# Attention, one expert layer and a gated FFN on one core: token numbers copied in FFN units, SP's order of a step, turn counts read by pairs, third row group used from unit 12

## The reference, cut to what matters

```python
def phi(x):
    proj = np.einsum('bhsd,df->bhsf', x, w_phi)
    proj = proj - np.max(np.abs(proj), axis=-1, keepdims=True)
    return np.concatenate([np.exp(proj), np.exp(-proj)], axis=-1)
# attention, batch 4, 8 heads, 576 positions, head size 64
kv = einsum(phi(k), v); z = sum(phi(k)); x = (phi(q) @ kv) / (phi(q) @ z + 1e-6)
# 2304 tokens of 512, top-1 of 8 experts, hidden 1024
e = argmax(x @ w_gate); y = gate_w * eom * (relu(x @ w1[e]) @ w2[e])
# gated FFN, hidden 1536
xn = y / sqrt(mean(y * y) + 1e-6) * rms_g
out = (silu(xn @ w_gate) * (xn @ w_val)) @ w_out
```

## Time and profile before

| | us |
|---|---|
| three runs | 873.22, 875.22, 879.47; median 875.22 |
| the profiled execution, its own time | 873.63 |
| span of its profile | 871.9 |
| PE busy | 840.2 (96% of the span) |
| DVE busy | 538.9 (62%) |
| ACT busy | 347.3 (40%) |
| POOL busy | 161.4 (19%) |
| mean granted TensorE clock | 0.998 of full speed |

### The profile page before, as it was taken

One profiled execution on the slowest core, in us unless ns is written; L12 is line 12 of the kernel. 1 busy time (PEld: TensorE's weight loads), 2 busy tenths in 40 slices (PEclk: granted clock), 3 DMA queues, 4 the chain that ended last, 5 costly groups with the idle time before them and its releaser, 6 DMA issues.

```text
span 871.9 us, 16594 instructions
## 1 busy us (share of the span) xinstructions
PE 840.2 (96%) x6216; PEld 757.3 (87%) x6217; DVE 538.9 (62%) x934; ACT 347.3 (40%) x547; POOL 161.4 (19%) x169
## 2 busy tenths in 40 slices
PE   8999999998988999999989999999999999999997
PEld 6685867767988999999989999999999998888885
DVE  5688786989766954445569777666765774212210
ACT  4544454573155533322354443333433443212211
POOL 1010302112350433203421031111110000101101
PEclk9999999999999999999999999999999999999999
DMA  8613713112349544554662852232421945343320
GB/s 285 209 57 138 275 54 108 55 38 75 127 175 267 227 114 97 141 148 150 184 230 77 280 180 79 79 80 79 142 71 54 357 150 184 123 139 125 125 101 36
DMA packets 65226, 122.41 MB, mean 140 GB/s; under 512 B 9200, under 2 KB 43120, under 8 KB 62480
## 3 DMA queue, kind: packets, MB, share of 16 engines
q1 hardware_dynamic: 57600, 91.98, 34.3%
q0 software_dynamic: 3488, 17.85, 5.3%
q10 hardware_dynamic: 4080, 11.80, 3.9%
HBM read 77.54 MB, written 44.09 MB: 139 GB/s over the span
## 4 chain that ended last, share of the span: by engine, by line
PE 78%; DVE 11%; issue 6%; DMA 2%; ACT 1%; DVEq 1%; SPq 0%; another core or an unknown queue 0%; POOLq 0%; POOL 0%; ACTq 0%
PE ps L1207 9%; PE ps L1209 9%; PE ps L1208 9%; PE ps L1259 5%; PE ps L1258 5%; PE ps L1260 5%; PE ps L956 3%; PE ps L1115 3%; PE ps L1116 3%; PE ps L1117 3%; PE ps L1128 3%; PE ps L1130 3%; PE ps L1129 3%; PE ps L1011 3%; PE ps L916 2%
## 5 line engine op out<-in xcount | busy, mean ns | idle before, releaser
L1207 PE MATMUL ps<-sH,tb 128*128 128x384 f32 x504 | 171.0, 339 | 5.9 <-DVE val L2018 2.9
L1208 PE MATMUL ps<-sL,tb 128*128 128x384 f32 x504 | 170.0, 337 | 0.0
L1209 PE MATMUL ps<-sH,tb 128*128 128x384 f32 x504 | 169.9, 337 | 0.0
L1207 PEld LDWEIGHTS ps<-sH,tb 128*128 128x128 f32 x504 | 95.0, 189 | 8.5 <-DVE val L2018 4.9
L1208 PEld LDWEIGHTS ps<-sL,tb 128*128 128x128 f32 x504 | 95.1, 189 | 0.1
L1209 PEld LDWEIGHTS ps<-sH,tb 128*128 128x128 f32 x504 | 95.2, 189 | 0.0
L2036 DVE TENSOR_TENSOR hTL<-h_st,hTH 128x768 fp32r<-128x768 f32 x36 | 33.0, 954 | 97.4 <-ACT hTH L1516 97.4
L1260 PE MATMUL ps<-woH,hTL 128*128 128x512 f32 x216 | 84.1, 389 | 0.0
L1259 PE MATMUL ps<-woL,hTH 128*128 128x512 f32 x216 | 84.1, 389 | 0.0
L1258 PE MATMUL ps<-woH,hTH 128*128 128x512 f32 x216 | 84.0, 389 | 0.0
L1115 PE MATMUL ps<-xmH,w1H 128*128 128x288 f32 x256 | 76.8, 300 | 5.9 <-issue 2.8
(11 more groups left out here) (246 smaller groups left out, 1784.8 us busy)
## 6 DMA issues: line engine op xcount, KB each, us to landing
h_dram<-hid SPq DMA_DIRECT2D x36, 384.0 KB, 2.8
h_st<-h_dram SPq DMA_DIRECT2D x18, 768.0 KB, 4.1
t_dram<-tb SPq DMA_DIRECT2D x6, 1792.0 KB, 5.7
t_raw<-in_ffn_up SPq DMA_DIRECT2D x13, 512.0 KB, 3.2
tb<-t_dram ACTq DMA_DIRECT2D x6, 1024.0 KB, 6.7
xin<-xs_dram SPq DMA_DIRECT2D x9, 578.2 KB, 9.3
xs_dram<-zrow SPq DMA_DIRECT2D x8, 578.2 KB, 7.9
qT<-in_q SPq DMA_DIRECT2D x4, 1152.0 KB, 5.8
```

The source lines that it names most:

```text
L1207: e.matmul(to, wh, xh, start=(fresh and c == 0), stop=False, skip_group_check=True)
L1208: e.matmul(to, wh, xl, start=False, stop=False, skip_group_check=True)
L1209: done = e.matmul(to, wl, xh, start=False, stop=(c == 1), skip_group_check=True)
```

## The change

1. **Token numbers.** The copies to `ids_dram` leave the steps of the expert stage. All eight are issued by SP in the FFN units 6, 8, ..., 20 (a loop in unit 21 takes further steps, of which there are none with these inputs). `idF` is read in unit 23 and not 15, `idI` made in unit 25 and not 17.
2. **SP's order of a step.** `rows_out` stands before `step_weights_in`.
3. **SP's order at the turn to the FFN.** `group_in(0)` comes before `operands_in(0)`; `operands_in(1)` waits for DVE's first copy of group 0 (`s_hi0`) and no more for PE's last hidden chunk. In unit 4 the last rows' store and `group_in(2)` stand before `hidden_out(4)`.
4. **Turn counts.** The two numbers of both turns are read at the pair's beginning; DVE reads the first TILES of the next pair there too.
5. **Third row group.** Visit 5 of groups 0 and 1 moves ahead; group 2 is first used at unit 12 and not 10. Its sums are made by DVE in units 9 "B", 10 "A" and 10 "B"; its splits move by two units. Visit 6's weights are split in unit 14 and not 13. Each group's sums have a semaphore of their own.

```diff
-MADE_AT = {6: 13, 7: 16, 8: 19, 9: 22, 10: 23, 11: 26}
-UNITS = ([(v, sg) for sg in range(2) for v in range(3)] + [(3, 0), (3, 1), (4, 0), (4, 1), (3, 2), (4, 2)]
-         + [(v, sg) for v in range(5, 9) for sg in range(NSG)]
+MADE_AT = {6: 14, 7: 16, 8: 19, 9: 22, 10: 23, 11: 26}
+UNITS = ([(v, sg) for sg in range(2) for v in range(3)] + [(v, sg) for v in range(3, 6) for sg in range(2)]
+         + [(v, 2) for v in range(3, 6)] + [(v, sg) for v in range(6, 9) for sg in range(NSG)]
...
+SUM_AT = {(1, "A"): ((1, 0), (1, 1)), (1, "B"): ((1, 2), (1, 3)), (9, "B"): ((2, 0), (2, 1)), (10, "A"): ((2, 2),),
+          (10, "B"): ((2, 3),)}
...
+NUMBERS_AT = tuple(range(6, 6 + 2 * (NTOK // G), 2))
...
-        def turn_of(e, x):
-
-            tiles = e.value_load(tab[0:1, bass.ds(x + TILES, 1)], min_val=0, max_val=NTOK // G)
-            first = e.value_load(tab[0:1, bass.ds(x + FIRST, 1)], min_val=0, max_val=NTOK // G + E)
-            return tiles, first
+        def turns_of(e, pair):
+
+            return [(e.value_load(tab[0:1, bass.ds(pair * 2 + (par + TILES), 1)], min_val=0, max_val=NTOK // G),
+                     e.value_load(tab[0:1, bass.ds(pair * 2 + (par + FIRST), 1)], min_val=0, max_val=NTOK // G + E))
+                    for par in range(2)]
...
             with e.Fori(0, pairs) as pair:
-                for par in range(2):
-                    tiles, first = turn_of(e, pair * 2 + par)
+                counts = turns_of(e, pair)
+                for par, (tiles, first) in enumerate(counts):
...
             with e.Fori(0, total - 2) as n:
                 rows_next(n + 2)
                 weights_out(n + 1)
+                rows_out(n, column_of(n))
                 step_weights_in(n + 2)
-                col, row = column_of(n), row_of(n)
-                rows_out(n, col)
-                numbers_out(n, col, row)
...
-            e.wait_ge(s["e_st"], 16 * 8)
-            operands_in(0)
             e.wait_ge(s["xst"], total * 16)
             settle(e, "carry_sp")
             group_in(0)
-            prior_col, prior_row = column_of(prior), row_of(prior)
-            rows_out(prior, prior_col)
-            e.wait_ge(s["pe_s1"], total * FC)
-            settle(e, "carry_sp")
+            e.wait_ge(s["e_st"], 16 * 8)
+            operands_in(0)
+            rows_out(prior, column_of(prior))
+            e.wait_ge(s["s_hi0"], 1)
             operands_in(1)
...
             for u in range(NU):
-                hidden_out(u)
                 if u == ROOT_AT + 1:
                     rows_out(last, last_col)
                     e.wait_ge(s["s_lo"], 7)
                     e.wait_ge(s["xst"], total * 16 + 32)
                     settle(e, "carry_sp")
                     group_in(2)
+                hidden_out(u)
...
-                if u == 8:
-                    numbers_out(prior, prior_col, prior_row)
-                if u == 10:
-                    numbers_out(last, last_col, last_row)
-                if u == 15:
-                    e.wait_ge(s["idst"], total * 16 + 16)
+                if u in NUMBERS_AT:
+                    n = NUMBERS_AT.index(u)
+                    if n > 0:
+                        e.wait_ge(s["idst"], n * 16)
+                    with nc.allow_non_contiguous_dma(reason="token numbers"):
+                        e.dma_start(ids_dram[bass.ds(column_of(n), G), :], xs_dram[bass.ds(row_of(n), G), DM:DM + 1])\
+                            .then_inc(s["idst"], 16)
...
             e.wait_ge(s["s_lo"], 7)
             add_squares(total - 1)
-            e.wait_ge(s["s_lo"], 14)
-            row_sums(2, 0)
-            row_sums(2, 1)
...
                 with e.Fori(0, pairs) as pair:
-                    for par in range(2):
-                        tiles, first = turn_of(e, pair * 2 + par)
-                        nxt = e.value_load(tab[0:1, bass.ds(pair * 2 + (par + TILES + 1), 1)], min_val=0,
-                                           max_val=NTOK // G)
+                    counts = turns_of(e, pair)
+                    after_pair = e.value_load(tab[0:1, bass.ds(pair * 2 + (TILES + 2), 1)], min_val=0, max_val=NTOK // G)
+                    for par, (tiles, first) in enumerate(counts):
+                        nxt = counts[1][0] if par == 0 else after_pair
...
             def beside(u, pos):
 
+                for sg, n in SUM_AT.get((u, pos), ()):
+                    row_sum(sg, n)
```

More of the change, by code:

```diff
@@ L307, in build_program @@
             "FFN up weights of a step: loaded, sums, operands split, stored": "e_in e_add e_hi e_lo e_st",
-            "FFN rows loaded (one per group), their sums, operands split": "x_in0 x_in1 x_in2 s_add s_add1 s_hi0 s_hi s_lo",
+            "FFN rows loaded (one per group), their sums, operands split": "x_in0 x_in1 x_in2 s_add0 s_add1 s_add2 s_hi0 s_hi s_lo",
             "FFN up operands loaded (two parts per buffer)": "t_a0 t_a1 t_a2 t_b0 t_b1 t_b2",
@@ L579, in rows_next, with numbers_out @@
                 rows_in(row)
-            def numbers_out(n, col, row):
-                e.wait_ge(s["idst"], n * 16 + 16)
+            def numbers_out(n):
+                e.wait_ge(s["idst"], n * 16)
                 settle(e, "carry_sp")
                 with nc.allow_non_contiguous_dma(reason="token numbers"):
-                    e.dma_start(ids_dram[bass.ds(col, G), :], xs_dram[bass.ds(row, G), DM:DM + 1])\
+                    e.dma_start(ids_dram[bass.ds(column_of(n), G), :], xs_dram[bass.ds(row_of(n), G), DM:DM + 1])\
                         .then_inc(s["idst"], 16)
@@ L669, in _ @@
             operands_in(2)
-            last_col, last_row = column_of(last), row_of(last)
+            last_col = column_of(last)
             for u in range(NU):
-                hidden_out(u)
                 if u == ROOT_AT + 1:
@@ L681, in _ @@
                         weights_in(vis)
-                if u == 8:
-                    numbers_out(prior, prior_col, prior_row)
-                if u == 10:
-                    numbers_out(last, last_col, last_row)
-                if u == 15:
-                    e.wait_ge(s["idst"], total * 16 + 16)
+                if u in NUMBERS_AT:
+                    n = NUMBERS_AT.index(u)
+                    if n > 0:
+                        e.wait_ge(s["idst"], n * 16)
+                    with nc.allow_non_contiguous_dma(reason="token numbers"):
+                        e.dma_start(ids_dram[bass.ds(column_of(n), G), :], xs_dram[bass.ds(row_of(n), G), DM:DM + 1])\
+                            .then_inc(s["idst"], 16)
+                if u == NUMBERS_AT[-1] + 1:
+                    with e.If(total > NTOK // G):
+                        with e.Fori(NTOK // G, total) as n:
+                            numbers_out(n)
+                if u == NUMBERS_AT[-1] + 3:
+                    e.wait_ge(s["idst"], total * 16)
                     settle(e, "carry_sp")
@@ L2099, in _ @@
                 beside(u, "C")
-                if u == 17:
+                if u == NUMBERS_AT[-1] + 5:
                     e.wait_ge(s["id_in"], 16)
```

62 lines of the change are left out of this document (26 added, 36 removed).

## The result

The changed kernel takes 879.83 us (median of 20 runs, 876.48 to 884.87). The kernel before, run beside it on the same chip, takes 876.86 us (20 runs, 873.22 to 879.72). The ratio is 1.0033, with a 95% interval of 1.0019 to 1.0047: about 3 us slower. That is within 1% as forecast, but on the other side of 1, and the time is over the range's end of 877.5. The profiled execution of the changed kernel has a span of 877.0 us.

The account below looks back on a forecast made before the run. PE, busy 191.0 of 198.8 us in the expert stage, leaves only gaps, some 9 us touched. Terms +2.2 + 1.5 - 1.8 - 4.0 + 2.0 - 1.5 + 0.2 = -1.4 from 873.6 give 872.2, stated as 872.0; range 866 to 877.5.

Parts of the forecast that it names:

- Part 4: FFN unit 4: its store, behind the rows' store and group 2's load, delays unit 6's sigmoid; +2.0 us.
- "very late" rival: Unit 4: rows' store held behind both ACT loads to about 502, unit 4's store lands near 512; 875.3 us, chance 0.13.
- The second landing: Unit 4's store, issued at 501.0 behind group 2's load, lands 9.2 us later, at 510.2.
- The upper bound: Unit 4's store: at most a 3.6 us gap of PE plus a fall of the clock.
- The rule that I weighed against the rows: DMA engines alternate between queue rows packet by packet, so unit 4's store would come in time; sum 2 us lower.
- Part 2: Expert steps: the rows' store goes out 3.7 us earlier, ending PE's 1.83 us wait for ACT's copy; -1.8 us.
- Part 3: Turn to the FFN: group 0's load first removes PE's 0.60 and most of 2.52 us, and the clock's fall; -4.0 us.
- Part 1: Expert stage: reading four counts at a pair's start lengthens two gaps by 1.44 us, removes 0.71 between turns; +2.2 us.
- The clock's fall behind the 3.1 us gap: First pair's start: a gap forecast at 3.0 us drops PE's clock to half; +1.5 us, chance 0.6.
- Part 5: FFN units 8 to 10: moving the third group's sums from POOL to DVE removes unit 9's 1.54 us gap; -1.5 us.
- Part 6: Smaller edits: unit 14's weight splits may delay ACT by some tenths, plus chance hits of POOL's sums; +0.2 us.
- the base: The profiled execution's own 873.6 us, from which the terms were counted; the three runs' median is 1.6 higher.

Follow-up runs that it names:

- f1: The changed kernel itself, measured again on another chip: 870.78 us against 870.04 before, ratio 1.0004.
- f2: The changed kernel with unit 4's store back ahead of the last rows' store and group 2's load, on f1's chip: 863.35 us, ratio 0.9922.
- e2: The kernel before with only unit 4's store moved behind the last rows' store and group 2's load: 882.71 us against 875.01, ratio 1.0089.
- e3: The kernel before with only both turns' counts read at a pair's start: 876.86 us against 875.01, ratio 1.0021.
- e8: The changed kernel with unit 4's store between SP's wait for the last rows' landing and group 2's load: 872.17 us against 878.28 before, ratio 0.9934.
- e11: The kernel before with only the token numbers' copies moved out of the expert steps, old order of rows' store and weights' load: 866.31 us, ratio 0.9955.
- e4: The kernel before with only the turn to the FFN changed (group 0 loaded first, second visit's operands later): 873.84 us against 875.01, ratio 0.9983.
- f3: The changed kernel with unit 4's store first and counts read turn by turn as before, on f1's chip: 863.86 us, ratio 0.9925.
- e1: The changed kernel with unit 4's store back ahead of the last rows' store and group 2's load: 869.25 us against 875.01 before, ratio 0.9932.

## Why the prediction was wrong

*Part 4, the store of unit 4, forecast +2.0, measured 7.4 (f1 against f2) and 7.7 (e2).* This is the step that failed: the chain of waits, its place and the instruction that waits were right, the size was not. The step that was wrong is "the store landed 6.4 us after its issue: 500.3". The 6.4 us of the earlier trace rows were taken as what the store needs, and kept while its issue moved 3.3 us forward. But it was mostly a wait for ACT's loads, whose time SP's order doesn't change. Before, ACT's second load was issued at 493.33 and the rows' store at 496.85, 3.5 us behind it; now the distance is 0.8 us (492.81 and 493.59), no packet of the store moved before 497.5, and it took 8.4 us. An issue 3.3 us earlier brought a landing only 1.2 us earlier (503.2 and 502.0), and the whole list behind it went out 1.7 us later than forecast. The four runs with unit 4's store behind the rows' store have 8.4 to 9.1 us there; of the other twelve runs and the kernel before, all have 6.1 to 7.4, but for e3's 9.7. With that unit 4's store landed at 512.1, which is the "very late" rival almost to the tenth, by its own reason (the rows' store held back behind ACT's loads to about 502); I gave it 0.13. The second landing, 9.2 us behind group 2's load, was right (9.4). And the rival itself was priced too low, with a gap of 3.6 (measured 4.19) and one fall of the clock of 1.5 us; the clock stayed at half for twice as long, which cost some 2.5. The upper bound should have been about 8, not 5.

What stands behind a load on SP's own queue waited for it: 9.4 us against 4.4 in e8. The rule that I weighed against the rows (Trainium skill, DMA: Bandwidth & Descriptors, "Queues, rings and completion order", queue rows take turns packet by packet) is about transfers of different queue rows, and spoke for the rows' store beside ACT's loads. The trace doesn't bear out what I drew from it: from 494.2 to 497.5 only ACT's queue moved packets, and both did from 497.5 on. Whether the engines had packets of the store to choose from in the first stretch, no view here shows.

*Part 2, forecast -1.8, measured -6.4.* A sized-down term again. I saw the wait at ACT's copy, but priced the number copies by who waits for them, and not by what they take from the others' transfers (3.9 us by e11, which also takes away the wait at ACT's copy without the new order). The rest, 2.4 us, would be the earlier store of the rows, but it is a difference of two chips' ratios whose intervals overlap, so that share isn't shown.

*Part 3, forecast -4.0, measured -1.5 alone and about 0 behind part 2.* The gap of 2.52 was caused by DVE's reading of the empty turn, which part 1 removes, not part 3. I had the reading in the text and booked it in the wrong part; for the sum of all parts it is the same. What was too high was the rest: the delay of the rows by group 1's later load was named as a bound and not put in. It made unit 1 longer by 0.9 to 1.0 us in the changed kernel and e4, though not in every execution: PE's gap there is 0.50 before, 1.3 to 1.6 in seven executions with the new order of SP's loads, 0.5 to 0.9 in four others.

*Part 1, forecast +2.2 and 1.5 for the clock.* Gaps 3.12 and 1.99 against 3.0 and 1.9; +1.8 alone (e3, with the reserve made there), and 0 in the changed kernel (f2 against f3) with the 2.2 at the turn. The clock's fall behind the 3.1 us gap, to which I gave 0.6, came in three of the six profiled executions that have that gap (e1, e8, f1; not in the changed kernel's first profile, e3 and f2).

*Part 5, forecast -1.5, measured -1.7,* within noise, and with the gap gone from the trace. *Part 6:* gaps of 0.3 us in unit 14 or 15, as forecast.

*The sum and its base.* The measured terms, each in the company of the others, are -6.4, 0, 0, +7.4 and -1.7: -0.7 us, where the forecast had -1.4, and the two measurements say +0.3 and +3 (the single terms are known to some 2 us each). That the sum comes near the forecast is luck: part 2 gained 4.6 more than forecast and part 4 cost 5.4 more, and parts 1 and 3 were 3.7 too dear and 4.0 too good. The time itself is 7.8 us above 872.0, and 3.2 of that is the base: the profiled execution and the three runs lay under what 20 runs of the kernel before gave, 876.86. On the chip of f1 the same kernel takes 870.78, inside the range; the time alone says little without the kernel before beside it.

A version that beats both kernels is f4: the changed kernel with the store first and the counts read in the turn, 861.29 us against 870.04 before and 870.78 changed, on one chip (ratio 0.9887).

## What to carry to other kernels

Before an issue is moved ahead of others on a queue, list what now stands behind it, and price the landing of each by a row in which it stands behind a transfer as large, not by its own earlier row. Ask of each landing what the transfer waited for: where other queues' loads were ahead of it, an earlier issue doesn't bring as early a landing. A DMA is priced twice, once by who waits for it and once by what it takes from transfers beside it; a copy of a thousand bytes in 4-byte pieces can be dear. Where a wait is named in the ledger of one edit, check which edit takes away what really ended it, since edits that share a gap don't add up.

## What the runs showed of the hardware

- The attention stage, the same code everywhere, ends at 210.5 to 210.9 us in seven profiled executions on two chips and at 215.7 to 215.9 in four on a third, all without a stretch at half clock in it; on a fourth chip, with one or two such stretches of 3.4 us, at 218.0 to 219.7. Chips thus differ by 5 us, 0.6% of the time, and the clock's falls in one execution add up to 3.4, each of the two as much as this change does in all, or more.
- A store of 576 KB that SP issued 0.8 us behind loads of 1024 and 768 KB from ACT's queue had no packet moved for 3.9 us; one of 384 KB behind SP's own load of 1536 KB had none for 5.7 us (changed kernel, to 497.5 and 508.4).
- Stretches at half clock lasted 3.4 us behind most gaps, 6.8 behind that of 4.19 and around f1's of 3.11, and 10.2 around e2's 7.75. Behind PE gaps of 2.2 to 2.5 at the turn they came in five of eight profiled executions, behind gaps of 3.1 in three of six, and behind the pair starts' 1.6 in none of eleven; two of the six gaps of 2.0 at a second pair's start had one (e8, f1). A table of gaps gives a chance of it, no certainty.
- Reading one table value costs ACT's queue 0.62 us and DVE's 0.72, so that DVE's five at a pair's start took 3.7 us in e1, from 241.9 to 245.6.
